# Attention, routed experts and a rational layer on one core: stage one reordered around the early gather, with its constants, fillers and weight splits moved

## The chip, the core and the metric

The kernel runs on one core of a Trainium2 chip. The core has a matrix engine (PE, TensorE; its weight loads are listed as PEld), a vector engine (DVE), a scalar engine (ACT), GpSimd (POOL), and SyncE (SP), which here only issues DMAs. The metric is the time of the program on the device in microseconds (us); lower is better.

## The reference, cut to what matters

Three layers follow each other.

1. **Decayed attention** (batch 2, 8 heads, 768 steps, head size 64): `state = gamma * state + k v^T; y = scale * q state`. Its output is read as `x`, 1536 tokens by 512.
2. **Routed experts** (8 experts, 512 to 1024 to 512, capacity 384 rows each): `logits = x @ w_gate`; each token goes to its `argmax` expert, at the next free position in arrival order; `h = max(x w1, 0)`, `y = h w2`, and the row is scaled by the softmax value of its expert.
3. **A rational layer** (512 to 2048 to 512): `h = x @ w_in`, `g = P(h) / (Q(h) + 1e-6)`, `out = g @ w_out`.

All is in single precision. The kernel gets this from a faster product by splitting each operand into a rounded high part and the rest ("split", H and L), and making three products of them.

## The kernel before, in words

**Stage one** handles 12 tiles of 128 tokens (`t` = 0 to 11, NT = 12; the first batch is t = 0 to 5). In `pe_tile(t)` PE transposes q and k of tile t+1, makes the gate products of tile t-1 (`pe_logits_apart`, `pe_logits_sum`), the state product, the row transposes (`pe_rows`), the query-state product, the scores of t+1, the positions of t-1 and last the values of t (`pe_values`). DVE in `dve_tile(t)` copies the gate sums, chooses the expert of each token (`dve_choose`), makes `tok_hot` (`dve_token`), turns the running count into a place (`dve_place`), masks the scores of t+1 (`dve_mask`), and at t = 6 to 9 takes one quarter of a weight split (`dve_split`, 128x1024). ACT copies results out of the banks and makes the high part of the split; POOL applies the decay tables; SP loads q, k, v three tiles ahead, stores each tile's rows to `xbuf` in memory (`store_x`) and loads weights. `pe_index(t)` adds a tile's tokens to the table of which token sits in which slot.

**The tail of stage one.** The first expert's rows must be in place before its first product. All but those of the last two tiles come by an early gather: once tile 9 is in the table, `dve_index0` copies the first 256 slots, and POOL issues two indirect DMAs from `xbuf` into `xd` (`pool_x_stored`). PE turns them (`pe_x_stored`, 8 products against the identity), and adds the rows of the last two tiles by products with a selection matrix (`pe_x_late(0)` and `(1)`, whose matrices come from `dve_fit`). ACT and DVE split the sum (`act_xH_first`, `dve_xL_first`), and `pe_up` of expert 0 starts. `act_gates` and `dve_gates` make the softmax values, which nothing needs before layer three. `pe_hold(n)` is n idle products of 128x128 on zeros.

**The experts and layer three** are long rows of products on PE, each weight matrix loaded (2 MB at a time) and split in turn.

The order on each engine is that of the code; engines meet only by semaphores. Each engine, and SP's list of DMAs, goes through its list in that order, and an instruction that waits holds up all behind it. The constants come as one table `cst` in four DMAs on ACT's queue, two under the semaphore `s_ident`, two under `s_cst`.

## Time and profile before

| what | us |
|---|---|
| median of 3 runs (lowest to highest) | 574.54 (572.18 to 575.68) |
| the profiled execution, its own time | 575.22 |
| its span in the trace | 573.4 |
| PE busy | 549.8 (96%) |
| DVE busy | 404.2 (70%) |
| ACT busy | 320.8 (56%) |
| stage one up to the first expert's product | 96.7 |

The span is cut by the hardware profiler around the engines' work; 1.8 us lie outside of it. In the profile a row names the line of the kernel, the engine, the operation and what it writes and reads.
### The profile page before, as it was taken

The numbers are of one execution on the slowest core, as the hardware profiler recorded it, in microseconds if no ns is written. First come the engines' busy times: TensorE is split into PE (matmuls) and PEld (weight loads), VectorE is DVE, ScalarE is ACT, GpSimd is POOL, SyncE is SP. The second block draws the span as 40 slices with busy tenths as digits, with TensorE's granted clock in tenths as the row PEclk, the third lists the DMA queues.
The fourth block names the chain that finished last, engine by engine and source line by source line (L and its number), as shares of the span: only waits on it lengthen the run. The fifth ranks groups of instructions, "written<-read, shape, count | busy, mean of one in ns | idle before, by whom it ended". The sixth has DMA issues, their size and how long they took to land.

```text
span 573.4 us, 9046 instructions
## 1 busy us (share of the span) xinstructions
PE 549.8 (96%) x3415; PEld 468.3 (82%) x3415; DVE 404.2 (70%) x718; ACT 320.8 (56%) x480; POOL 56.1 (10%) x55
## 2 busy tenths in 40 slices
PE   8999868999999999999958999999999999999997
PEld 6887757998989989989736888888888888888885
DVE  3567764745647457464758988888888888888885
ACT  3546421635646446454856757565775755756553
POOL 3424311101001011000050000100000000000000
PEclk9999998999999999999978999999999999999999
DMA  9999749367994583853040000100100000100001
GB/s 218 274 241 276 217 154 346 123 248 245 417 376 174 200 290 137 304 201 130 37 114 1 1 19 19 37 2 0 75 18 19 0 2 1 74 0 1 0 1 74
DMA packets 63871, 72.64 MB, mean 127 GB/s; under 512 B 39890, under 2 KB 40402, under 8 KB 63827
## 3 DMA queue, kind: packets, MB, share of 16 engines
q1 hardware_dynamic: 58706, 60.06, 31.6%
q0 software_dynamic: 2240, 7.34, 4.1%
q10 hardware_dynamic: 2880, 4.66, 2.2%
q8 instruction: 27, 0.44, 0.3%
q14 instruction: 18, 0.14, 0.1%
HBM read 59.20 MB, written 12.85 MB: 126 GB/s over the span
## 4 chain that ended last, share of the span: by engine, by line
PE 89%; DVE 4%; DMA 2%; ACT 2%; issue 1%; POOL 0%; POOLq 0%; DVEq 0%
PE bank L755 26%; PE bank L757 25%; PE bank L756 25%; PE bank L252 2%; PE bank L275 1%; DMA xd<-xbuf,index 1%; PE bank L286 1%; PE bank L719 1%; PE bank L1020 1%; DVE T L689 1%; PE bank L320 1%; PE bank L236 1%; DMA x2n<-ybuf,slot_all 1%; DVE atm L408 1%; PE bank L304 1%
## 5 line engine op out<-in xcount | busy, mean ns | idle before, releaser
L689 DVE TENSOR_TENSOR T<-raw,T 128x1024 fp32r<-128x1024 f32 x64 | 77.1, 1232 | 54.9 <-ACT T L683 54.6
L755 PE MATMUL bank<-x2H,T 128*128 128x512 f32 x192 | 76.8, 400 | 3.6 <-DVE pa L1108 2.2
L1078 ACT ACTIVATE sq<-bank 128x512 f32<-128x512 f32 x48 | 28.7, 597 | 86.1 <-PE bank L757 85.9
L757 PE MATMUL bank<-x2H,T 128*128 128x512 f32 x192 | 75.6, 394 | 0.0
L756 PE MATMUL bank<-x2L,T 128*128 128x512 f32 x192 | 75.5, 393 | 0.0
L755 PE MATMUL bank<-T,gL 128*128 128x512 f32 x192 | 74.8, 390 | 0.0
L757 PE MATMUL bank<-T,gH 128*128 128x512 f32 x192 | 74.7, 389 | 0.0
L756 PE MATMUL bank<-T,gH 128*128 128x512 f32 x192 | 74.7, 389 | 0.0
L755 PE MATMUL bank<-xH,T 128*128 128x256 f32 x256 | 72.5, 283 | 1.6 <-DVE xL L750 1.6
L756 PE MATMUL bank<-xL,T 128*128 128x256 f32 x256 | 72.5, 283 | 0.0
L757 PE MATMUL bank<-xH,T 128*128 128x256 f32 x256 | 72.5, 283 | 0.0
L683 ACT ACTIVATE T<-raw 128x1024 fp32r<-128x1024 f32 x64 | 65.2, 1058 | 4.6 <-ACT ysb L814 3.6
L1097 DVE SCALAR_TENSOR_TENSOR wa<-sq,coef,wa 128x512 f32<-128x512 f32 x48 | 36.0, 750 | 39.8 <-ACT wa L1080 39.8
L755 PEld LDWEIGHTS bank<-xH,T 128*128 128x128 f32 x256 | 49.1, 192 | 2.1 <-issue 1.8
L755 PE MATMUL bank<-T,hL 128*128 128x512 f32 x128 | 50.7, 396 | 0.0
L757 PE MATMUL bank<-T,hH 128*128 128x512 f32 x128 | 49.9, 390 | 0.0
L756 PE MATMUL bank<-T,hH 128*128 128x512 f32 x128 | 49.8, 389 | 0.0
L756 PEld LDWEIGHTS bank<-xL,T 128*128 128x128 f32 x256 | 49.1, 192 | 0.3
L757 PEld LDWEIGHTS bank<-xH,T 128*128 128x128 f32 x256 | 49.1, 192 | 0.0
L755 PEld LDWEIGHTS bank<-x2H,T 128*128 128x128 f32 x192 | 36.6, 191 | 12.1 <-issue 3.0
L757 PEld LDWEIGHTS bank<-x2H,T 128*128 128x128 f32 x192 | 36.5, 190 | 7.9
L756 PEld LDWEIGHTS bank<-x2L,T 128*128 128x128 f32 x192 | 36.6, 191 | 7.4
(139 smaller groups left out, 1023.0 us busy)
## 6 DMA issues: line engine op xcount, KB each, us to landing
raw<-in_moe_w_dram SPq DMA_DIRECT2D x14, 2048.0 KB, 10.5
raw<-in_moe_w_dram SPq DMA_DIRECT2D x8, 512.0 KB, 4.9
ybuf<-ysb ACTq DMA_DIRECT2D x16, 256.0 KB, 5.4
w_in_raw<-in_moe_w_in_dram SPq DMA_DIRECT2D x2, 2048.0 KB, 18.5
raw<-in_moe_w_out_dram SPq DMA_DIRECT2D x4, 1024.0 KB, 9.2
qin<-in_q_dram SPq DMA_DIRECT2D x12, 256.0 KB, 5.2
kin<-in_k_dram SPq DMA_DIRECT2D x12, 256.0 KB, 4.7
vin<-in_v_dram SPq DMA_DIRECT2D x12, 256.0 KB, 5.1
```

Source lines behind the costliest of these rows:

```text
L236: last = e.transpose(bank[0][:, p * P:(p + 1) * P], qs[t % 2][:, p * P:(p + 1) * P], ident)
L252: last = e.matmul(bank[2 + r][:, p * P:(p + 1) * P], kT[t % 2][rows, p, :], qT[t % 2][rows, p, :], start=True, stop=True)
L275: e.matmul(bank[4][:, p * P:(p + 1) * P], state[(t - 1) % 2][:, p, :], qT[t % 2][:, p, :], start=p == 0, stop=False, skip_group_check=True)
L286: last = e.matmul(bank[4][r * D:(r + 1) * D, p * P:(p + 1) * P], vs[t % 2][:, h * D:(h + 1) * D], atm[t % 2][:, r, p, :], start=t % C == 0 ...
L304: e.matmul(bank[7][:, 0:E], lgT[:, :], pick[:, :], start=True, stop=True).then_inc(s_lg, 1)
L683: e.activation(W[w][:, 0, cols], raws[par][:, w, cols], ACT.Copy).then_inc(r.wH[w], 1)
L689: e.tensor_tensor(W[w][:, 1, cols], raws[par][:, w, cols], W[w][:, 0, cols].bitcast(F32), ALU.subtract).then_inc(r.wL[w], 1)
L755: nc.tensor.matmul(out_, aL, bH, start=start, stop=False)
L756: nc.tensor.matmul(out_, aH, bL, start=False, stop=False)
L757: return nc.tensor.matmul(out_, aH, bH, start=False, stop=stop)
L1078: e.activation(sq[o][:, :], h[:, :], ACT.Square).then_inc(s_w, 1)
L1097: e.scalar_tensor_tensor(out=wa[n % 2][:, :], in0=sq[n % 2][:, :], scalar=coef[:, 5:6], in1=wa[n % 2][:, :], op0=ALU.mult, op1=ALU.add).th ...
```

## The change

- `dve_split` in stage one moves from the end of `dve_tile` (behind the mask) to between `dve_token` and `dve_place`.
- Tail on PE: the table product of tile 9 stands before the values of tile 10, not after them; that of tile 10 goes to the end. The positions of tile 10 come after the values of tile 11. `pe_x_late(0)` stands before `pe_x_stored` and starts the accumulation.
- Tail on DVE: `dve_index0` stands in tile 10 right behind `dve_place(9)`, before the mask of tile 11. In the last tile `dve_fit(1)` stands before `tok_hot`, `lane_hot` and `tok`.
- The first expert's split (`act_xH_first`, `dve_xL_first`) stands before the gate computations.
- SP: the 2 MB load of expert 1's first matrix moves from t = 9 to behind the last `store_x`, which itself waits for the early gather.
- Constants: three DMAs on ACT's queue (identity, decay tables, causal mask) and one on SP's behind the first six loads; `before` and `ones` are computed on DVE; the small tables are made behind the first two masks.
- Fillers: 8 to 5 at the start, 3 to 2 and 1 in the tail; the last 6 stay.

```diff
@@ dve_tables
-            e.wait_ge(s_cst, 16 * 2)
-            e.tensor_copy(before[:, :], cc("before")).then_inc(s_const, 1)
-            e.tensor_copy(ones[:, :], cc("ones")).then_inc(s_const, 1)
+            e.tensor_tensor(before[:, :], causal, ident, ALU.subtract).then_inc(s_const, 1)
+            e.memset(ones[:, :], 1.0).then_inc(s_const, 1)
...
+            e.wait_ge(s_cst, 16)
@@ dve_place(t, last=False)
             e.tensor_scalar(inside[:, :], step_no[:, :], step_of[:, :], None, ALU.is_equal).then_inc(s_in, 1)
+            if last:
+                dve_fit(1)
+                dve_token(t)
@@ pe_first_tile
-            pe_hold(8)
+            pe_hold(5)
@@ pe_tile
-            if t >= 2:
+            if t >= 2 and t != NT - 1:
                 pe_index(t - 2)
...
             if t + 1 < NT:
                 pe_scores(t + 1)
-            pe_positions(t - 1)
+                pe_positions(t - 1)
+                if t == NT - LAST:
+                    pe_index(t - 1)
             pe_values(t)
@@ pe_last_tiles
-            pe_index(NT - 2)
-            pe_hold(3)
+            pe_positions(NT - 2)
+            pe_hold(2)
             pe_logits(NT - 1)
             pe_rows(NT - 1)
+            pe_x_late(0)
+            pe_positions(NT - 1)
+            pe_hold(1)
             pe_x_stored()
-            pe_positions(NT - 1)
-            pe_x_late(0, False)
-            pe_x_late(1, True)
+            pe_x_late(1)
+            pe_index(NT - 2)
             pe_index(NT - 1)
@@ dve_tile
                 dve_token(t - 1)
+                if SPLIT_FROM < t <= SPLIT_FROM + WC:
+                    dve_split(main, 0, 0, 0, t - SPLIT_FROM - 1)
                 dve_place(t - 1)
+                if t == NT - LAST:
+                    dve_index0()
             if t + 1 < NT:
                 dve_mask(t + 1)
-            if SPLIT_FROM < t <= SPLIT_FROM + WC:
-                dve_split(main, 0, 0, 0, t - SPLIT_FROM - 1)
@@ sync
+            e.dma_start(cst[:, lay["kdecay"][1]:CW], consts[:, lay["kdecay"][1]:CW]).then_inc(s_cst, 16)
             e.wait_ge(s_zm, 2)
...
-                if t == NT - 3:
-                    sp_weights(main, 0, 1, 0)
             e.wait_ge(main.xd, 16 * NMAIN)
             store_x(NT - 1)
+            sp_weights(main, 0, 1, 0)
@@ scalar
             act_rows(NT - 1)
+            act_xH_first()
             act_gates()
@@ vector
             dve_first_q()
+            e.wait_ge(s_causal, 16)
+            dve_mask(0)
+            dve_tile(0)
             dve_tables(e)
...
             dve_fit(0)
             dve_choose(NT - 1)
-            dve_token(NT - 1)
-            dve_place(NT - 1)
-            dve_fit(1)
+            dve_place(NT - 1, True)
             dve_index()
+            dve_xL_first()
```

The next lists show the order of instructions on an engine at three places. `[waits ...]` names semaphores. First DVE in tile 6 of stage one, from `tok_hot` of tile 5 to the copy of the next gate sums. `T<-raw,T` is the split, `junk` and `cum` open the place computation, `atm` is the mask, and `lgT` is the copy that PE's gate sum waits for. Before:

```order
L443 TENSOR_SCALAR tok_hot<-hot_all,row_no 128x8 [waits s_hot]
L449 SCALAR_TENSOR_TENSOR junk,pt_all<-bank,hot_all 128x8 [waits s_ps]
L451 TENSOR_TENSOR cum<-cum,hot_all 128x8
L453 TENSOR_SCALAR junk,step_of<-step_at,pt_all 128x3 [waits s_pc]
L456 SCALAR_TENSOR_TENSOR lane_of<-step_of,pt_all 128x1 [waits s_so]
L458 TENSOR_SCALAR inside<-step_no,step_of 128x3
L461 TENSOR_SCALAR lane_hot<-cst,lane_of 128x128 [waits s_im,s_lo]
L464 TENSOR_TENSOR tok<-tok_hot,inside 128x24 [waits s_th,s_in]
L408 TENSOR_TENSOR atm<-bank,cst 128x512 [waits s_y,s_sc]
L408 TENSOR_TENSOR atm<-bank,cst 128x512
L689 TENSOR_TENSOR T<-raw,T 128x1024 [waits main_w1H]
L422 COPY lgT<-bank 128x128 [waits s_lg,s_la]
```

Now, the same place:

```order
L443 TENSOR_SCALAR tok_hot<-hot_all,row_no 128x8 [waits s_hot]
L698 TENSOR_TENSOR T<-raw,T 128x1024 [waits main_w1H]
L449 SCALAR_TENSOR_TENSOR junk,pt_all<-bank,hot_all 128x8 [waits s_ps]
L451 TENSOR_TENSOR cum<-cum,hot_all 128x8
L453 TENSOR_SCALAR junk,step_of<-step_at,pt_all 128x3 [waits s_pc]
L456 SCALAR_TENSOR_TENSOR lane_of<-step_of,pt_all 128x1 [waits s_so]
L458 TENSOR_SCALAR inside<-step_no,step_of 128x3
L464 TENSOR_SCALAR lane_hot<-cst,lane_of 128x128 [waits s_im,s_lo]
L467 TENSOR_TENSOR tok<-tok_hot,inside 128x24 [waits s_th,s_in]
L408 TENSOR_TENSOR atm<-bank,cst 128x512 [waits s_y,s_sc]
L408 TENSOR_TENSOR atm<-bank,cst 128x512
L422 COPY lgT<-bank 128x128 [waits s_lg,s_la]
```

The split stood in front of `lgT`; it now stands in front of `junk`, which waits for PE's positions (`s_ps`).

Second, PE at the end of tile 10: positions of tile 9 (L328, L329), values of tile 10 (L286), the table product (L341) and the gate product of tile 10 (L297). Before:

```order
L328 MATMUL bank<-hot_all,before 128x8 [waits s_lc,s_cum,s_hot]
L329 MATMUL bank<-cum,ones 128x8
L286 MATMUL bank<-atm,vs 64x128 [waits s_xT,s_mk,s_vs]
L286 MATMUL bank<-atm,vs 64x128 x7
L341 MATMUL bank<-tok,lane_hot 128x24 [waits s_se,s_ix]
L297 MATMUL bank<-xT,wg 32x128 [waits s_pc,s_xT]
```

Now:

```order
L328 MATMUL bank<-hot_all,before 128x8 [waits s_lc,s_cum,s_hot]
L329 MATMUL bank<-cum,ones 128x8
L341 MATMUL bank<-tok,lane_hot 128x24 [waits s_se,s_ix]
L286 MATMUL bank<-atm,vs 64x128 [waits s_xT,s_mk,s_vs]
L286 MATMUL bank<-atm,vs 64x128 x7
L297 MATMUL bank<-xT,wg 32x128 [waits s_pc,s_xT]
```

The table product, which waits for the end of `dve_place(9)` (`s_ix`), is now ahead of the values, and they wait behind it.

Third, PE from the last tile's row transposes (L320) on: L351 (L350 now) is `pe_x_stored`, L365 `pe_x_late`, L601 (L608) the count per expert, L222 a filler. Before:

```order
L320 MATMUL bank<-cst,xT 128x128 [waits s_x,s_xT]
L320 MATMUL bank<-cst,xT 128x128 x3
L351 MATMUL bank<-cst,xd 128x128 [waits s_mk,main_xd]
L351 MATMUL bank<-cst,xd 128x128 x7
L328 MATMUL bank<-hot_all,before 128x8 [waits s_lc,s_cum,s_hot]
L329 MATMUL bank<-cum,ones 128x8
L365 MATMUL bank<-fit,xt 128x256 [waits s_fit,s_x]
L365 MATMUL bank<-fit,xt 128x256 x3
L365 MATMUL bank<-fit,xt 128x256 [waits s_fit,s_x]
L365 MATMUL bank<-fit,xt 128x256 x3
L341 MATMUL bank<-tok,lane_hot 128x24 [waits s_ix]
L601 MATMUL bank<-cum,ones 128x8 [waits s_pc,s_cum]
```

Now:

```order
L365 MATMUL bank<-fit,xt 128x256 [waits s_mk,s_fit,s_x]
L365 MATMUL bank<-fit,xt 128x256 x3
L328 MATMUL bank<-hot_all,before 128x8 [waits s_lc,s_cum,s_hot]
L329 MATMUL bank<-cum,ones 128x8
L222 MATMUL bank<-zero 128x128
L350 MATMUL bank<-cst,xd 128x128 [waits main_xd]
L350 MATMUL bank<-cst,xd 128x128 x7
L365 MATMUL bank<-fit,xt 128x256 [waits s_mk,s_fit,s_x]
L365 MATMUL bank<-fit,xt 128x256 x3
L341 MATMUL bank<-tok,lane_hot 128x24 [waits s_index0,s_ix]
L341 MATMUL bank<-tok,lane_hot 128x24 [waits s_ix]
L608 MATMUL bank<-cum,ones 128x8 [waits s_pc,s_cum]
```

One of the two late products and the last positions now stand ahead of the wait for the gather (`main_xd`).

## Rows read from the trace of the kernel before

**Rows 1.** The chain that ended last, by engine, share of the span.

```profile
PE 89%; DVE 4%; DMA 2%; ACT 2%; issue 1%; POOL 0%; POOLq 0%; DVEq 0%
```

**Rows 2.** That chain in time, first 9 us: start us, us, what (x records).

```profile
3.54 3.41 PE bank L222 x16
6.96 0.62 PE bank L236 x4
...
8.83 1.16 PE bank L252 x16
```

**Rows 3.** Instructions in time, first 14 us: start us, us, engine, line [idle before].

```profile
5.11 0.69 DVE L532 TENSOR_TENSOR qs<-qin,cst 128x512 f32<-128x512 f32 x1 [2.46 <-DMA cst<-consts_dram]
...
11.97 1.04 POOL L532 TENSOR_TENSOR qs<-qin,cst 128x512 f32<-128x512 f32 x1 [0.41 <-DMA qin<-in_q_dram]
...
13.92 0.66 PE L236 MATMUL bank<-cst,qs 128*128 128x128 f32 x4
```

**Rows 4.** Stretches from:to: us, busy of PE, PEld, DVE, ACT, POOL, PEclk, DMA.

```profile
6.00:8.00 2.00, 2.00 (x13) 1.76 (x12) 0.70 (x6) 0.40 (x1) 0.43 (x1) 1.00 1.23 278
...
86.00:87.00 1.00, 0.81 (x4) 0.81 (x5) 0.00 (x0) 0.00 (x0) 0.00 (x0) 0.50 0.03 10
```

**Rows 5.** PE in time, tiles 7 to 10: gate sums that waited.

```profile
51.37 0.39 PE L304 MATMUL bank<-pick,lgT 128*128 128x8 f32 x2 [0.64 <-DVE lgT L422]
...
65.62 0.39 PE L304 MATMUL bank<-pick,lgT 128*128 128x8 f32 x2 [1.55 <-DVE lgT L422]
```

**Rows 6.** DVE and POOL in time, 42 to 72 us.

```profile
42.66 0.17 DVE L449 SCALAR_TENSOR_TENSOR junk<-bank,hot_all 128x8 f32<-128x8 f32 x1 [1.26 <-PE bank L329]
...
47.73 0.17 DVE L449 SCALAR_TENSOR_TENSOR junk<-bank,hot_all 128x8 f32<-128x8 f32 x1 [0.36 <-PE bank L329]
...
56.55 2.13 POOL L532 TENSOR_TENSOR qs<-qin,cst 128x512 f32<-128x512 f32 x1
...
63.49 1.87 DVE L689 TENSOR_TENSOR T<-raw,T 128x1024 fp32r<-128x1024 f32 x1
...
70.82 1.21 DVE L689 TENSOR_TENSOR T<-raw,T 128x1024 fp32r<-128x1024 f32 x1
```

**Rows 7.** The chain in time, end of stage one.

```profile
91.66 1.97 PE bank L365 x8
...
96.72 0.35 PE bank L755
```

**Rows 8.** Instructions in time, 75 to 95 us.

```profile
75.22 1.09 PE L286 MATMUL bank<-atm,vs 128*64 128x128 f32 x16
...
76.43 0.19 PE L341 MATMUL bank<-tok,lane_hot 128*128 128x24 f16 x1
...
77.49 0.15 DVE L484 CAST index<-bank 128x2 uint32<-128x2 f32 x1
...
77.89 0.39 PE L304 MATMUL bank<-pick,lgT 128*128 128x8 f32 x2 [0.45 <-DVE lgT L422]
...
79.78 1.09 PE L286 MATMUL bank<-atm,vs 128*64 128x128 f32 x16
...
79.92 0.95 POOL L709 DMA_INDIRECT xd<-xbuf,index  x1 [0.30 <-issue]
...
81.26 0.60 DVE L477 TENSOR_SCALAR fit<-cst,lane_of,mine 128x128 f32<-128x128 f32 x2
...
86.19 3.42 PE L351 MATMUL bank<-cst,xd 128*128 128x128 f32 x16 [2.82 <-DMA xd<-xbuf,index]
...
93.52 1.58 PE L222 MATMUL bank<-zero 128*128 128x128 f32 x12
```

**Rows 9.** The tile xd: landing of its 16 gathers, from their issue.

```profile
DMA to landing us min/median/max: 4.1/7.2/7.8
```

**Rows 10.** ACT in time: splits of expert 1's first matrix.

```profile
109.97 3.90 ACT L683 ACTIVATE T<-raw 128x1024 fp32r<-128x1024 f32 x4
```

More of the change, by code:

```diff
@@ L170, in build_program @@
         s_ident, s_cst, s_par, s_zm, s_const = (sem(n) for n in ("s_ident", "s_cst", "s_par", "s_zm", "s_const"))
-        s_wg, s_q0, s_xz, s_la, s_lt = (sem(n) for n in ("s_wg", "s_q0", "s_xz", "s_la", "s_lt"))
+        s_wg, s_q0, s_xz, s_la, s_lt, s_causal = (sem(n) for n in ("s_wg", "s_q0", "s_xz", "s_la", "s_lt", "s_causal"))
         s_index0, s_mine, s_fit, s_x0 = (sem(n) for n in ("s_index0", "s_mine", "s_fit", "s_x0"))
@@ L347, in pe_x_stored @@
             e.wait_ge(main.xd, NMAIN * 16)
-            e.wait_ge(s_mk, 2 * NT)
             for kk in range(KD):
@@ L351, in pe_x_stored @@
                     last = e.matmul(x_bank(kk)[:, s * P:(s + 1) * P], xd[:, s, kk * P:(kk + 1) * P], ident,
-                                    start=kk % 2 + s == 0, stop=False, skip_group_check=True)
+                                    start=False, stop=False, skip_group_check=True)
             last.then_inc(main.xt, NMAIN)
@@ L356, in x_bank, with pe_x_late @@
             return bank[2 + kk // 2][:, kk % 2 * NMAIN * P:(kk % 2 + 1) * NMAIN * P]
-        def pe_x_late(i, last_one):
+        def pe_x_late(i):
             e = nc.tensor
@@ L363, in pe_x_late @@
             e.wait_ge(s_fit, NMAIN * (i + 1))
+            e.wait_ge(s_mk, 2 * NT)
             for kk in range(KD):
                 last = e.matmul(x_bank(kk), xt[t % 2][:, kk * P:(kk + 1) * P], fit[i][:, :, :].rearrange("p a b -> p (a b)"),
-                                start=False, stop=True, skip_group_check=True)
-                if last_one and kk % 2:
+                                start=i == 0 and kk % 2 == 0, stop=i == LAST - 1, skip_group_check=True)
+                if i == LAST - 1 and kk % 2:
                     last.then_inc(s_x0, 1)
@@ L443, in dve_token, with dve_place @@
             e.tensor_scalar(tok_hot[t % 2][:, :], hot_all[:, t, :], row_no[:, t:t + 1], None, ALU.mult).then_inc(s_th, 1)
-        def dve_place(t):
+        def dve_place(t, last=False):
             e = nc.vector
@@ L859, in step @@
                     stored()
-            if split:
-                act_xH_first()
-            else:
+            if not split:
                 act_first_split(r)
@@ L877, in step @@
                         dve_split(r, *following(i, par), 0, c)
-            if split:
-                dve_xL_first()
-            else:
+            if not split:
                 for c in range(WC):
@@ L1347, in _ @@
         def _(e):
-            for a, b, s in ((0, lay["ident"][1], s_ident), (lay["qdecay"][0], lay["kdecay"][1], s_ident),
-                            (lay["ident"][1], lay["qdecay"][0], s_cst), (lay["kdecay"][1], CW, s_cst)):
+            for a, b, s in ((lay["ident"][0], lay["ident"][1], s_ident), (lay["qdecay"][0], lay["kdecay"][1], s_ident),
+                            (lay["causal"][0], lay["causal"][1], s_causal)):
                 e.dma_start(cst[:, a:b], consts[:, a:b]).then_inc(s, 16)
@@ L1394, in _ @@
             e.wait_ge(s_const, 6)
-            dve_mask(0)
-            for t in range(NT - 1):
+            for t in range(1, NT):
                 dve_tile(t)
-            dve_index0()
-            dve_tile(NT - 1)
             dve_fit(0)
             dve_choose(NT - 1)
-            dve_token(NT - 1)
-            dve_place(NT - 1)
-            dve_fit(1)
+            dve_place(NT - 1, True)
             dve_index()
+            dve_xL_first()
             e.wait_ge(s_cnt, 1)
```

## The prediction, on record before the change was run

> **What bounds the kernel now.** I read the chain of waits by engine first: PE holds 89% of it [rows 1], and from the first expert's product at 96.72 on it is one row of products, so what is taken off before 96.72 comes off the end one for one. The same chain in time order shows what PE does at the start: it sits in its own fillers [rows 2]. PE's instructions in time with their idle time show four late gate sums in tiles 7 to 10 [rows 5], and the tail shows PE waiting for the gather and then for the last split [rows 7, 8]. So there are three places, and I cost each. The profiled execution took 575.22 us, 0.7 above the median of the three runs, so the sum is made against 575.22.
>
> **Start.** 16 filler records take 3.41 us, 0.213 each [rows 2]; three fillers are six records, 1.28 us, and the rest would end at 5.68. The first decayed q is ready at 5.11 + 0.69 = 5.80 [rows 3], so the transposes could begin at 5.85 and not at 6.96: 1.1 us. PE's products still have the slow length there (the first of the transposes was the last slow one), so the 8 transposes up to 8.83 lose what they had as fast ones, about 0.4 to 0.5 us. The small tables on DVE are six operations, 0.70 us together [rows 4]; they stood in idle time and now stand between the second mask and PE's first gate product, beside PE's transposes of tile 2, 0.66 us for a group of four [rows 3]; I take 0.1 for what sticks out. The part of the constants that moves to SP is one more issue ahead of q of tile 2. Before, POOL waited 0.41 us for that q and was done at 13.01, and PE used it at 13.92 [rows 3]: 0.9 us of room, which the earlier start uses up, but there are also two tables fewer to fetch. I take **0.5 us** gained; the ends are 1.1 (all of it) and -0.3 (q of tile 2 late by one issue, and none of the filler time kept).
>
> **Middle.** PE waited for `lgT` four times behind a split: 0.64, three such waits, and 1.55 once [rows 5], 3.47 us in all. The split now fills the time in which DVE waits for the positions. In a full tile that is 1.26 us [rows 6], and a split is 1.21 [rows 6]: it fits, with no more than 0.05 to spare, in three tiles. In tile 6, which has no query-state product, the wait is only 0.36 [rows 6]. There the split pushes place and mask by 1.21 - 0.36, some 0.8 us, and they are next late for `lgT` of the following tile; before, the whole 1.21 stood there and made 0.64, so about 0.25 us is left. Gain 3.47 - 0.25 = **3.2 us**. The long wait of 1.55 belongs to a split that took 1.87 [rows 6]. In two other tiles POOL's decay took 2.13 beside the split [rows 6], where its others take 1.04 as in [rows 3]: the two disturb each other, and either can be the one that loses. In the new place POOL's decays are over, so I let the whole 1.55 go. The GPSIMD Engine Reference of the Trainium skill (section "Specifications") says that GpSimd shares its SBUF interfaces with VectorE and that vector instructions with two SBUF inputs contend; the trace agrees, by those 2.13 and 1.87. Ends: 3.5, and 1.6, where the 0.91 of excess comes back and 0.3 remains in each of the other tiles.
>
> **Tail,** in the times of the trace before. The table product of tile 9 stood at 76.43 and took 0.19 [rows 8]; the values of tile 10 now come behind it, at 76.62 and not 75.22: **1.4 us later**. From these values to the next was 79.78 - 75.22 = 4.56; the wait of 0.45 for `lgT` behind the mask [rows 8] mostly goes, since PE comes later: 4.1. So the values of tile 11 start at 80.7 and end at 81.8 (1.09). The positions of tile 10, which stood just ahead of them, are now behind. From the positions to the end of `fit` was 81.86 - 79.7 = 2.1 to 2.2 [rows 8]: 84.0. Until then PE has two fillers, the logits and the rows. Then `pe_x_late(0)`, 1.97 [rows 7], to 86.0, the positions and one filler to 86.5, and `pe_x_stored` can start, against 86.19 before: **0.3 later**.
>
> The gather need be there only then. Its copy of the index came at 77.49; it now follows the table product at once, at 76.7, 0.8 sooner, and the second gather, issued at 79.92 before [rows 8] and landed just ahead of PE's start at 86.19, 6.2 us later, is issued at 79.1. At that it lands at 85.3, at the longest of the sixteen, 7.8 [rows 9], at 86.9. The wait is about gone, whichever way. The 2 MB load ahead of it was no hindrance that I count, so I give its move nothing.
>
> `pe_x_stored` took 3.42 for 16 records, 0.214 each, at half the clock [rows 4, 8]; fillers at full clock take 1.58 / 12 = 0.13 [rows 8]. PE had been idle 2.8 us before it; that idle time is now filled, so I take 2.3 and not 3.42: **1.1 gained**. Behind it stood positions and `pe_x_late(0)`, 91.66 - 89.61 = **2.05, gone from there**. `pe_x_late(1)` then starts at 88.8.
>
> From the start of `pe_x_late(1)` to the first product was 96.72 - 91.66 = 5.06 [rows 7], with DVE's gate computations in between. Now the split follows at once: the sum ends 1.97 later, the index copy and the first low part need about 1.0 more, and PE's own last fillers end at 95.10 - 91.66 = 3.44 [rows 8]. The fillers are the later: 3.5 with the extra table product, **1.55 gained**. Tail: -0.3 + 1.1 + 2.05 + 1.55 = 4.4; I take **4.3**. The ends are 2.9 (the gather at its longest and `pe_x_stored` still at half clock) and 4.9.
>
> What is late next: the gate computations run on DVE during expert 0's first products, some 2 us of work in front of a split of its second matrix, which is needed only when all products of the first are made. Expert 1's first matrix is split on ACT from 109.97 on [rows 10], now some 4 us sooner, at 105.6; its load, issued at about 87, has over 18 us. Nothing there costs anything as long as that holds.
>
> **Sum:** 0.5 + 3.2 + 4.3 = 8.0 us; 575.22 - 8.0 = **567.2 us**.
>
> **Rivals.**
>
> *The split is not hidden.* The margin is 0.05 us in a wait of 1.26, and tile 6 has none. If each split still delays place, mask and `lgT` by 0.5 us on PE, the middle gives 1.0 and not 3.2: 569.4. Against it: 1.21 was measured beside nothing of POOL's, and that is how it will run. Chance 0.12.
>
> *The tail gives half.* The values of tile 10 wait behind the table product for DVE's place, and all that hangs on them moves. If that chain costs 2 us more than I have, or the gather lands as late as before for another reason, the tail gives 2 us: 569.5 to 570.5. For it: I have moved this chain over five instructions that wait for each other, and each term of it was read from another order of work. Chance 0.15.
>
> *The load behind the gather starves expert 1.* Three loads of 2 MB now leave one after the other, with expert 1's two gathers among them. If these took over 11 us, 3 more than the longest [rows 9], PE would wait at expert 1; 2 to 5 us, 569 to 572. Chance 0.04.
>
> *Slower: the half clock.* At the start and in the tail PE gets fewer fillers and a new wait of 1.1 us in front of the table product. The trace shows 0.50 granted right after an idle time of 2.8 us [rows 4, 8]. If the clock is at half from the table product to the first expert's products, `pe_x_stored` keeps its 1.1, the two late products take some 2 more, the other 7 us of PE work in the tail 3.5 more, the expert's first products 1.5, and a start that stays slow 2: 10 us against a gain of 8, **577**. It decides against the change from 8 us of such losses on. TensorE: Matmul & The Clock Gate of the Trainium skill (part 1, "The HAM clock gate") says that the throttled clock is the default and only activity releases it, which speaks against taking fillers away. By that rule this case is the likelier the emptier PE gets. The rows have PE fuller in the tail than before, so I give it 0.05.
>
> **The numbers.** Forecast 0.60 (565.5 to 569.0 by itself), the rivals 0.36, unforeseen 0.04. The lower ends of the terms, -0.3 + 1.6 + 2.9 = 4.2, give 571.0; the upper, 1.1 + 3.5 + 4.9 = 9.5, give 565.7. With 0.5 us for the spread of a median of such runs the range is 565.0 to 571.5; outside of it are the half clock, part of the starving and little else. A difference under 1%, 5.7 us, can hardly be told from none here; faster by more than that means under 568.8. The forecast nearly all lies there, the first two rivals hardly: faster 0.62, same 0.32, slower 0.06.
>
> **What would show it.** Right: no wait of PE for `lgT` in tiles 8 to 10 and about 0.25 in tile 7; every split at 1.2; `pe_x_stored` at about 2.3 us with a granted clock of 1.00, starting within 0.5 us of the end of its filler; the first expert's product at 88.5 to 89 on the trace's own time, right behind the last filler. Wrong: splits at 1.9, idle time of PE in front of `pe_x_stored`, 0.50 granted anywhere between 76 and 90, a wait of POOL for q of tile 2 of over 1 us, or PE idle at the start of expert 1.

## The result and the profile after

| | median us (lowest to highest, executions) | against the kernel before of the same session |
|---|---|---|
| before | 573.95 (572.18 to 576.63, 20) | |
| the change | 570.62 (566.47 to 573.37, 20) | 0.9932 (0.9913 to 0.9952) |

The change is 3.3 us faster, 0.7%. The profiled execution took 570.54 us, its span is 568.7, against 575.22 and 573.4. The forecast was 567.2 in a range from 565.0 to 571.5: the time is inside, but well under half of the forecast gain of 8.0 is there (4.7 us between the two profiled executions, 3.3 between the medians). The executions of the change spread over 6.9 us, those of the kernel before over 4.5 here and over 7.7 and 7.9 us in two later sessions of measurement, so it is not shown that the change spreads more.

**Where the time went.** These are the starts of PE's tiles (`pe_transpose_qk`) and the first product of expert 0, read from PE's instructions in time:

| | tile 2 | tile 6 | tile 7 | tile 8 | tile 9 | tile 10 | first product |
|---|---|---|---|---|---|---|---|
| before | 19.87 | 43.58 | 48.65 | 55.32 | 61.99 | 69.58 | 96.72 |
| the change | 20.06 | 43.77 | 48.84 | 58.31 | 64.27 | 70.23 | 91.12 |

(`pe_tile(n)` begins with the transposes of tile n+1; that is the time given.) The start lost 0.2. Tile 7 took 9.47 instead of 6.67 and gave back what tiles 8 (5.96 for 6.67), 9 (5.96 for 7.59) and 10 gained. So the positions of tile 9, which PE computes in tile 10, come at 75.03, and came at 75.08 before. From there to the first product it is 16.1 instead of 21.6, 5.55 us shorter. Of the 5.6 at the first product 5.5 are left at the last copy of the output (564.68 for 570.16) and 4.7 in the span, since the last rows took 0.8 longer to land.

Start of the change, instructions in time (start us, us, engine, line, operation, [idle before, releaser]); it answers to [rows 2, 3]:

```profile
6.21 0.63 PE L236 MATMUL bank<-cst,qs 128*128 128x128 f32 x4 [0.74 <-DVE qs L535]
...
8.10 1.16 PE L252 MATMUL bank<-qT,kT 64*128 64x128 f32 x16 [0.83 <-ACT kT L376]
...
13.90 1.04 POOL L535 TENSOR_TENSOR vs<-vin,cst 128x512 f32<-128x512 f32 x1 [0.91 <-PE bank L236]
13.92 1.04 DVE L206 TENSOR_SCALAR step_at<-cst 128x3 f32<-128x3 f32 x1
...
14.88 0.16 DVE L207 TENSOR_SCALAR step_no<-cst 128x3 f32<-128x3 f32 x1
...
15.13 0.43 PE L297 MATMUL bank<-xT,wg 128*32 128x128 f32 x8 [0.85 <-issue]
```

The scores begin at 8.10 and not 8.83: 0.73 gained. Then one of the small tables, 128 by 3, takes 1.04 us, where its twin of the same form and size takes 0.16 right behind. It began 0.02 us after POOL's decay and ended with it. PE's first gate product waits 0.85 for these tables (in the kernel it waits for `s_const`, which the last of them completes; the profile names no releaser).

Tile 7 in time: VectorE, then POOL, then PE:

```profile
47.47 1.22 DVE L698 TENSOR_TENSOR T<-raw,T 128x1024 fp32r<-128x1024 f32 x1
48.60 0.16 DVE L449 SCALAR_TENSOR_TENSOR junk<-bank,hot_all 128x8 f32<-128x8 f32 x1
...
49.14 1.02 DVE L458 TENSOR_SCALAR inside<-step_no,step_of 128x3 f32<-128x3 f32 x1
50.08 1.14 DVE L464 TENSOR_SCALAR lane_hot<-cst,lane_of 128x128 f16<-128x128 f32 x1
```

```profile
49.07 1.06 POOL L535 TENSOR_TENSOR vs<-vin,cst 128x512 f32<-128x512 f32 x1 [3.03 <-PE bank L286]
50.10 1.04 POOL L535 TENSOR_TENSOR qs<-qin,cst 128x512 f32<-128x512 f32 x1
```

```profile
51.37 0.19 PE L341 MATMUL bank<-tok,lane_hot 128*128 128x24 f16 x1 [1.43 <-DVE tok L467]
...
52.76 0.48 PE L304 MATMUL bank<-pick,lgT 128*128 128x8 f32 x2 [0.24 <-DVE lgT L422]
53.10 1.10 PE L320 MATMUL bank<-cst,xT 128*128 128x128 f32 x4
53.99 1.92 PE L275 MATMUL bank<-qT,state 128*128 128x128 f32 x8
```

The split is hidden, as forecast, and pushes the start of `dve_place` from 47.73 [rows 6] to 48.60, as forecast. What was not forecast: `inside` and `lane_hot` now meet POOL's two decays and take 1.02 and 1.14 where they take 0.22 and 0.28 in another tile (43.40 and 43.53). The row that PE waits for, `tok`, is late by that, and PE stands for 1.43 us. Stretches of one us (from:to, us, busy of PE, PEld, DVE, ACT, POOL, granted clock of PE, DMA share, GB/s):

```profile
50.00:51.00 1.00, 0.00 (x0) 0.00 (x0) 1.00 (x2) 0.68 (x2) 1.00 (x2) 1.00 0.80 236
51.00:52.00 1.00, 0.63 (x13) 0.42 (x15) 1.00 (x4) 0.00 (x0) 0.14 (x1) 1.00 1.04 304
...
53.00:54.00 1.00, 1.00 (x7) 1.00 (x7) 0.61 (x4) 0.35 (x1) 0.00 (x0) 0.50 0.94 213
54.00:55.00 1.00, 1.00 (x6) 1.00 (x6) 0.93 (x4) 0.76 (x2) 0.00 (x0) 0.50 1.14 262
55.00:56.00 1.00, 1.00 (x7) 0.78 (x5) 0.77 (x1) 0.78 (x1) 0.00 (x0) 0.50 0.52 160
```

Behind that wait 0.50 is granted, 1.2 GHz, from 53 to 56: the transposes L320 take 1.10 instead of 0.64, the query-state product 1.92 instead of 1.06. That is some 1.6 us on top of the wait. "TensorE: Matmul & The Clock Gate" of the Trainium skill (part 1) says that idle stretches of PE bring the throttled level back. These rows agree, with 0.50 behind a wait of 1.43, though waits in other tiles and runs did not bring it, as the experiments show.

The tail in time; it answers to [rows 7, 8]:

```profile
76.38 0.19 PE L341 MATMUL bank<-tok,lane_hot 128*128 128x24 f16 x1 [1.14 <-DVE tok L467]
76.50 1.09 PE L286 MATMUL bank<-atm,vs 128*64 128x128 f32 x16
...
78.29 0.43 PE L297 MATMUL bank<-xT,wg 128*32 128x128 f32 x8 [0.70 <-ACT xT L383]
...
79.06 0.95 POOL L718 DMA_INDIRECT xd<-xbuf,index  x1 [0.31 <-issue]
79.13 0.39 PE L304 MATMUL bank<-pick,lgT 128*128 128x8 f32 x2 [0.41 <-DVE lgT L422]
...
84.03 1.97 PE L365 MATMUL bank<-fit,xt 128*128 128x256 f32 x8
...
86.19 1.95 PE L350 MATMUL bank<-cst,xd 128*128 128x128 f32 x16
...
87.97 1.89 PE L365 MATMUL bank<-fit,xt 128*128 128x256 f32 x8
```

No wait in front of the gathered rows' product (L350), which takes 1.95 at a clock of 1.00 where it took 3.42 [rows 8]. The three waits of 1.14, 0.70 and 0.41 came with the new order. In this execution the clock held behind them.

### The profile page after: what moved, and what is told of

Read it like the earlier page. It is cut to its first block, busy times and chain, and to the rows that moved or that the text cites. A ratio compares the mean times of both kernels' runs of the same rounds, so it can differ in the third digit from the quotient of the medians.

```text
span 568.7 us, 9034 instructions
## 1 busy us (share of the span) xinstructions
PE 548.0 (96%) x3409; PEld 466.8 (82%) x3409; DVE 405.7 (71%) x718; ACT 321.9 (57%) x480; POOL 54.0 (9%) x55
## 4 chain that ended last, share of the span: by engine, by line
PE 92%; DVE 2%; DMA 2%; ACT 2%; issue 1%; POOL 0%; POOLq 0%; ACTq 0%; DVEq 0%
PE bank L764 26%; PE bank L766 26%; PE bank L765 26%; PE bank L252 2%; PE bank L286 2%; PE bank L275 2%; PE bank L236 1%; PE bank L728 1%; PE bank L320 1%; PE bank L1025 1%; PE bank L266 1%; DMA x2n<-ybuf,slot_all 1%; DMA cst<-consts_dram 1%; PE bank L241 1%; PE bank L304 1%
```

## The experiments

The theory after the two traces. **One:** a VectorE operation on SBUF data that begins beside POOL's decay is held until that ends, and the edits at the start and in tile 6 push short operations there. **Two:** the waits that this and the new tail give PE let the granted clock fall, in some executions here, in others there, and that takes back part of the gain. The main rival to both: the tail's new order is simply worth less than the trace of one execution shows.

The expectations below number their own theories, and "theory one" in them is not always One here. All medians below are also given against the kernel before of the same session (medians 575.2, 575.18 and 574.74 in the three sessions; 573.95 beside the change). The kernel before itself moves by 1.25 us between sessions, and the intervals are 2 to 5 us wide, so differences of 1 to 2 us between two experiments are not shown by the medians alone; for these the traces are read.

**e1_tail_only: the tail's part alone on the kernel before.** Start, constants and the place of the split are undone:

```diff
@@ dve_tile, of the change
-                if SPLIT_FROM < t <= SPLIT_FROM + WC:
-                    dve_split(main, 0, 0, 0, t - SPLIT_FROM - 1)
                 dve_place(t - 1)
...
                 dve_mask(t + 1)
+            if SPLIT_FROM < t <= SPLIT_FROM + WC:
+                dve_split(main, 0, 0, 0, t - SPLIT_FROM - 1)
@@ pe_first_tile
-            pe_hold(5)
+            pe_hold(8)
```

> Only the tail of the change on the kernel before: order on PE and DVE at the end of stage one, load of expert 1 behind the gather, split of the first rows ahead of the gate computations; splits of tiles 6 to 9, constants and the first 8 fillers as before. My theory (the tail gives all of the gain, and start and middle cancel out in sum): from the positions of tile 9 to the first product of expert 0 it takes 16.1 us as with the whole change and not 21.6; first product at 91.2, time 5.5 us under the kernel before, ratio 0.990. Rival (the tail's gain needs the PE time that the middle freed or lost): under 3 us.

Measured: 571.64 us (569.08 to 572.07), 3.6 below before, ratio 0.9925 (0.9899 to 0.9952). That is neither the 5.5 of the expectation nor the under 3 of its rival. First product at 92.73, 4.0 before the old 96.72. The same three waits stand in the tail, and here the clock falls behind them:

```profile
79.00:80.00 1.00, 0.73 (x4) 0.73 (x5) 0.31 (x2) 0.00 (x0) 0.80 (x1) 0.52 0.53 78
80.00:81.00 1.00, 1.00 (x6) 1.00 (x5) 0.85 (x5) 0.15 (x1) 0.15 (x1) 0.50 0.55 209
81.00:82.00 1.00, 1.00 (x7) 1.00 (x6) 0.23 (x1) 0.44 (x1) 0.00 (x0) 0.50 0.50 160
```

So the tail by itself makes about what the whole change makes, and in this execution it carries a loss of its own.

**e2_split_only: the place of the split alone on the kernel before.**

```diff
@@ dve_tile, of the kernel before
                 dve_token(t - 1)
+                if SPLIT_FROM < t <= SPLIT_FROM + WC:
+                    dve_split(main, 0, 0, 0, t - SPLIT_FROM - 1)
                 dve_place(t - 1)
```

> Only the move of the four splits between tok_hot and place, on the kernel before. My theory: tiles 8 to 10 lose their waits for lgT (0.64 + 1.55 + 0.64 = 2.8 us gained), but in tile 7 the place computation of tile 5, pushed by 0.9 us, runs beside POOL's decays; inside and lane_hot take about 1.0 and 1.1 us instead of 0.2 and 0.3, PE waits 1.4 us for tok, and the clock falls to half for some 3 us. Tile 7 then is 9.4 us and not 6.7: sum 0 (ratio 1.000, within 0.002). Rival A (as predicted before: tile 6 costs 0.25 only): 3.2 us gained, 0.994. Rival B (the half clock comes from the fillers taken away at the start): tile 7 waits 1.4 but stays at full clock, 1.8 us gained, 0.997.

Measured: 572.45 us (569.95 to 573.88), 2.8 below before, ratio 0.9933 (0.9905 to 0.9962). The expectation of no gain was wrong. The three later tiles take 5.96 each, as forecast. Tile 7 takes 7.0: `inside` 1.02 beside POOL's first decay, `lane_hot` only 0.27, since POOL's second decay waited for its q until 51.18. PE waited 0.56 and the clock held in this tile. (It fell later, behind the old wait for the gather, here 3.09 us long, for 6.8 us; before it was 3.4 us behind 2.82. So the first product of this execution is only 1.8 us earlier.) The middle is worth nearly its 3.2 where only one of the two operations is held and the clock stays up. The two gains, 3.6 and 2.8, don't add up to the change's 3.3. The product of their ratios is 0.9859, against 0.9932 (0.9913 to 0.9952) measured for the change.

**e3_split6_back and e4_split6_tables: the split of tile 6 back behind the mask; and the small tables ahead of the first tile's choice too.**

```diff
@@ dve_tile
-                if SPLIT_FROM < t <= SPLIT_FROM + WC:
+                if SPLIT_FROM + 1 < t <= SPLIT_FROM + WC:
                     dve_split(main, 0, 0, 0, t - SPLIT_FROM - 1)
...
                 dve_mask(t + 1)
+            if t == SPLIT_FROM + 1:
+                dve_split(main, 0, 0, 0, 0)
@@ VectorE's list, e4 only
             dve_mask(0)
+            dve_tables(e)
             dve_tile(0)
-            dve_tables(e)
```

> The whole change, with the split of tile 6 alone put back behind the mask (tiles 7 to 9 keep the new place). My theory: tile 7 is 6.7 us again, its gate sum waits 0.64 for lgT, and no half clock there: 2.8 us less than the whole change, about 8.3 less than before, ratio 0.9865 against 0.9932. Rival (the three others would show the same conflict with POOL, or the half clock comes from elsewhere): the same time as the whole change, 0.993.

> As the run before, and the small tables are made between the first and the second mask (DVE and POOL idle there), not behind the second, where step_at took 1.04 us beside POOL's decay and PE's first gate product waited 0.85. My theory: that wait is gone, tile 2 starts at 19.1 to 19.2 and not at 20.06; 0.85 us less than the run before, ratio 0.985. Rival (the table of constants that now comes on SP's queue lands after 11 us and holds the second mask up): nothing gained or a loss of up to 1 us, with DVE waiting for the DMA of cst.

Measured: e3 571.46 us (567.83 to 572.55), 3.7 below before, 0.992 (0.9888 to 0.9952); e4 569.42 (566.55 to 573.45), 5.8 below, 0.9892 (0.9845 to 0.9938). Both are less than the expectations, 0.9865 and 0.985; e3 is nearer to its rival of no gain, and the intervals of e3, e4 and the change overlap. In e3 tile 7 is 6.67 again and the first product comes at 90.54, but the same collision has moved to tile 8, where it costs nothing, and to tile 9, which takes 6.99 us. VectorE and, below it, POOL:

```profile
57.94 1.11 DVE L432 SCALAR_TENSOR_TENSOR rankv<-lg_all,mx_all,cst 128x8 f32<-128x8 f32 x1
...
61.36 1.02 DVE L458 TENSOR_SCALAR inside<-step_no,step_of 128x3 f32<-128x3 f32 x1
```

```profile
57.98 1.04 POOL L535 TENSOR_TENSOR qs<-qin,cst 128x512 f32<-128x512 f32 x1 [1.60 <-DMA qin<-in_q_dram]
61.30 1.05 POOL L535 TENSOR_TENSOR vs<-vin,cst 128x512 f32<-128x512 f32 x1 [2.27 <-PE bank L286]
```

In e4 PE's wait for the tables is gone: from the first scores to tile 2 it takes 11.04 us, as in the kernel before, and 11.83 in e3. Tile 2 itself begins at 19.50 and at 19.66 in e3, hardly earlier, because the first transposes of this execution took 1.09 and not 0.63. Both show half clock in the tail, e3 for 3.4 us, e4 for 6.8:

```profile
75.00:76.00 1.00, 0.32 (x8) 0.20 (x8) 0.36 (x1) 0.60 (x1) 0.98 (x1) 0.85 0.00 0
76.00:77.00 1.00, 0.59 (x10) 0.26 (x3) 0.29 (x1) 0.00 (x0) 0.69 (x2) 0.50 0.28 45
...
81.00:82.00 1.00, 1.00 (x13) 0.67 (x9) 0.00 (x0) 0.05 (x1) 0.00 (x0) 0.50 0.00 0
```

**e5_tail_fill: e4, with fillers where PE waits in the tail.** This is the direct test of Two.

```diff
@@ pe_tile, of e4
                 pe_positions(t - 1)
                 if t == NT - LAST:
+                    pe_hold(4)
                     pe_index(t - 1)
...
+            if t == NT - 1:
+                pe_hold(2)
             pe_logits_apart(t - 1)
             if t % C < C - 1:
                 pe_state(t)
+            if t == NT - 1:
+                pe_hold(1)
             pe_logits_sum(t - 1)
```

> The kernel of e4_split6_tables with seven fillers (128x128, about 0.21 us each) put where TensorE waited in the tail: four ahead of the table product of tile 9, two ahead of the gate product of tile 10 and one ahead of its sum; the waits there were 1.14, 0.70 and 0.41 us. Theory one, the half clock decides: the holes of 1.1 and 0.7 us are what lets the granted clock fall to 0.50 between 75 and 83 us in e4 (7 us long). With fillers the clock stays 1.00 there, each product keeps its time of full clock, and the first product of expert 0 comes about 1.5 to 2.5 us earlier (89 instead of 91.1); median 567.0 to 568.0, against 569.4. Theory two, the clock falls for another reason or where the half clock lies costs nothing on the path: fillers change nothing, or cost what they overshoot (0 to 0.3 us); median 569.4 to 569.8.

Measured: **567.12 us (566.86 to 568.39)**, 8.1 below before, ratio 0.9879 (0.9849 to 0.991). First product at 87.80 instead of 91.11; no stretch below full clock before the experts; the spread is 1.5 us instead of e4's 6.9. PE in time, and stretches of two us:

```profile
73.07 0.19 PE L341 MATMUL bank<-tok,lane_hot 128*128 128x24 f16 x1
73.19 1.09 PE L286 MATMUL bank<-atm,vs 128*64 128x128 f32 x16
74.21 0.71 PE L222 MATMUL bank<-zero 128*128 128x128 f32 x4
74.98 0.42 PE L297 MATMUL bank<-xT,wg 128*32 128x128 f32 x8
75.33 0.49 PE L222 MATMUL bank<-zero 128*128 128x128 f32 x2
75.82 0.39 PE L304 MATMUL bank<-pick,lgT 128*128 128x8 f32 x2
```

```profile
74.00:76.00 2.00, 1.95 (x22) 1.20 (x19) 0.95 (x3) 0.60 (x1) 1.37 (x2) 1.00 0.00 0
76.00:78.00 2.00, 2.00 (x22) 1.88 (x23) 1.18 (x6) 0.60 (x1) 0.70 (x1) 1.00 0.63 164
```

By the medians, seven fillers of no use to the result make the kernel 2.3 us faster. By the ratios, against the kernel before of each session, it is 0.7 us, with overlapping intervals of six executions each, so the size is open. The cause can be read more firmly. First in the traces, by the time from the start of tile 10 to the first product of expert 0:

| | waits in the tail | half clock in it, us | from tile 10 to the first product |
|---|---|---|---|
| before | old order, 2.82 for the gather | 3.4 | 27.14 |
| e1, e3, e4 | 1.14, 0.70, 0.41 | 3.4, 3.4, 6.8 | 23.06, 22.47, 23.49 |
| the change, e6, e8 | 1.14, 0.70, 0.41 | 0 | 20.89, 20.88, 20.88 |
| e5, e10 | filled | 0 | 20.88, 20.89 |

The fillers themselves cost nothing, and the half clock costs 1.6 to 2.6 us where it comes. That also answers the main rival: the new order is worth what the trace of the change shows wherever the clock holds. Second, each execution has a mean granted clock on record, in which 3.4 us at half clock are 0.003. (Every profiled execution, before and after, has another 10.2 or 13.7 us of half clock near 290 us, so the mean is not of the tail alone.) Without the fillers (the change, e1, e3, e4) it is 0.985 or less in 17 of 46 executions; with them (e9, e12, e10, e5) in 1 of 25. Two holds for the tail. The clock is not all of the spread, though: the 9 executions of the change at 0.990 or more have a median of 568.81 and the 11 others of 571.38, and 4.3 us of spread are left within the first group.

**e6_pool_short: the whole change, POOL's decay of tiles 6 to 10 on 2 of 8 heads** (the rest is left out).

```diff
@@ pool_decay and decayed, of the change
-            decayed(e, t, 2).then_inc(s_vs, 1)
+            decayed(e, t, 2, 2 if 6 <= t <= 10 else H).then_inc(s_vs, 1)
```

> The whole change, with POOL's decay of q and v cut to 2 of its 8 heads in tiles 6 to 10 (the rest keeps what the buffer held, so part of the result is left out): POOL's tensor_tensor there falls from 1.04 to some 0.3 us. Theory one, VectorE's short operations are held for as long as a POOL operation runs beside them: in tile 7 the operations inside (1.02) and lane_hot (1.14) fall back to about 0.22 and 0.28, the wait of 1.43 us ahead of the row that waits for tok goes to 0.2 or less, tile 7 takes 6.0 us instead of 9.5 and tiles 8 to 10 stay at 6.0; the profiled run then stands 3 us better by the first product of expert 0 (88), and the median falls by 0.5 to 3 us, by how many executions had the half clock there. Theory two, those two operations are slow by their own kind or place in the row: they stay at 1.0 and 1.1 us, the wait stays, and the median stays at 570.6.

Measured: 569.45 us (567.37 to 573.55), 5.7 below before, 0.9913 (0.9881 to 0.9944). POOL and VectorE in the same tile:

```profile
49.12 0.42 POOL L535 TENSOR_TENSOR vs<-vin,cst 128x128 f32<-128x128 f32 x1 [3.66 <-PE bank L286]
```

```profile
49.20 0.38 DVE L458 TENSOR_SCALAR inside<-step_no,step_of 128x3 f32<-128x3 f32 x1
49.49 0.27 DVE L464 TENSOR_SCALAR lane_hot<-cst,lane_of 128x128 f16<-128x128 f32 x1
```

The edit shortened `vs` alone (the decay of q kept its 8 heads, contrary to what the expectation says), and that suffices here: `inside` ends within 0.05 us of POOL's end again, now after 0.38. PE's wait for `tok` is gone (0.24 for `lgT` is left), and the tile takes 6.36. `lane_hot` met no decay in this execution, since POOL's second waited for its q until 50.70, so this run tests `inside` alone. Theory one of the expectation holds: the length of the hold-up is what is left of POOL's operation. Other runs say the same: `row_no` (128 by 12) began 0.17 us behind a decay of 1.04 in e3 and took 0.90, and 0.20 us behind one in e10 and took 0.86, 0.16 alone. The gain in the median, 1.2 us under the change, is within the noise.

**e7_two_inputs: the whole change, `inside` and `lane_hot` in the form with a second SBUF input.**

```diff
@@ dve_place, of the change
-            e.tensor_scalar(inside[:, :], step_no[:, :], step_of[:, :], None, ALU.is_equal).then_inc(s_in, 1)
+            e.scalar_tensor_tensor(out=inside[:, :], in0=step_no[:, :], scalar=step_of[:, :], in1=ONES,
+                                   op0=ALU.is_equal, op1=ALU.mult).then_inc(s_in, 1)
```

(`ONES` stands for a slice of the table of ones; `lane_hot` likewise. The third DMA of the constants is made longer, to fetch that table.)

> The whole change, with inside and lane_hot made by scalar_tensor_tensor with a second input (a table of ones in SBUF) instead of tensor_scalar, same sizes (128x3 and 128x128). If the hold-up beside POOL's decay belongs to the one-input form tensor_scalar, the new ones take 0.25 and 0.35 us beside it and tile 7 takes 6.0 us; the median falls by 0.5 to 3 us. If any VectorE operation that begins beside POOL's decay is held, they take 1.0 to 1.1 us where they meet it, as before, tile 7 takes 9.5 (7 where the clock holds) and the median is 570.6 or 0.1 us more per tile for the longer form (571.5).

Measured: 571.36 us (568.56 to 575.81), 3.8 below before, 0.9949 (0.992 to 0.9978). VectorE, then POOL:

```profile
49.49 1.01 DVE L458 SCALAR_TENSOR_TENSOR inside<-step_no,step_of,cst 128x3 f32<-128x3 f32 x1
50.42 0.34 DVE L466 SCALAR_TENSOR_TENSOR lane_hot<-cst,lane_of 128x128 f16<-128x128 f32 x1
...
50.78 1.28 DVE L408 TENSOR_TENSOR atm<-bank,cst 128x512 f32<-128x512 f32 x2
```

```profile
49.42 1.06 POOL L538 TENSOR_TENSOR vs<-vin,cst 128x512 f32<-128x512 f32 x1 [3.02 <-PE bank L286]
50.76 1.04 POOL L538 TENSOR_TENSOR qs<-qin,cst 128x512 f32<-128x512 f32 x1 [0.27 <-DMA qin<-in_q_dram]
```

The hold-up does not hang on the one-input form. `lane_hot` fell between the two decays here and took 0.34, so PE waited 0.63, the clock held, and the tile took 7.07. And the mask, which began 0.02 us after POOL's second decay, kept its 1.28: one of its two inputs comes from PSUM.

**e8_bulk_back: the whole change, the bulk load back at t = NT - 3.**

```diff
@@ SP's list, of the change
+                if t == NT - 3:
+                    sp_weights(main, 0, 1, 0)
             e.wait_ge(main.xd, 16 * NMAIN)
             store_x(NT - 1)
-            sp_weights(main, 0, 1, 0)
```

> The whole change, with the bulk load of expert 1's weights back in tile 9 of the loop on SP's queue (sp_weights at t = NT - 3) instead of behind the wait for the gather. Theory one (that of the prediction): the load's place costs and gives nothing; the gather lands by its own latency of 3.4 to 8.2 us, TensorE does not wait for it, and the median stays at 570.6 (570.0 to 571.2). Theory two: the load beside the gather delays its rows; the stored rows' product at 86 us then waits 1 to 3 us, expert 0 begins that much later, median 571.6 to 573.6.

Measured: 570.67 us (568.46 to 571.87), 4.5 below before, 0.9922 (0.9891 to 0.9953). The median is that of the change (570.62), the intervals overlap, and PE does not wait in front of the gathered rows' product (86.64, right behind its filler): no worth of the load's place shows. Tile 7 again has the wait of 1.43 and half clock behind it (9.46 us).

**e9, e10 and e12: the same fillers on the whole change, on e3 and on e1. e11: e5 with four fillers ahead of expert 0 instead of six** (`pe_hold(6)` to `pe_hold(4)` in `pe_last_tiles`).

> The whole change, nothing undone, with the seven fillers of e5_tail_fill in the tail's waits. Theory one: the place of the split in tile 6 and the half clock there are a loss of their own (tile 7 at 9.5 us in the profiled run of the change, 7.0 where the clock holds), the tail's half clock another. The fillers take away only the second: median 568.0 to 569.5, between the change (570.6) and e5 (567.1), and the profile shows tile 7 at 7 to 9.5 us and no half clock after 70 us. Theory two: the tail's half clock was all of it, and the split's place costs nothing in most executions: median 567.1 to 567.6.

> The kernel of e5_tail_fill with the constant tables back behind the first tile's choice on VectorE (as in the change), so that only their place differs from e5. Theory one, the tables' place costs what the gate product of tile 1 waits in the profiles (0.7 to 0.85 us, 1.7 in one): median 567.7 to 568.2. Theory two, the later rows absorb it (TensorE waits for the choice in every tile): median 567.0 to 567.3.

> The kernel of e5_tail_fill with four fillers instead of six ahead of expert 0's first product. In e5 the six end at 87.80 while xL's first half is written by 87.4 at the latest: two fillers fewer bring the first product 0.3 to 0.4 us earlier, median 566.7 to 566.8 (theory one). Rival: the product then waits for the second half of xL (written at about 88.0), and nothing is gained: 567.1.

> The kernel before with the change of the tail alone (that of e1_tail_only) and the seven fillers in its waits. Theory one: the new order of the tail is worth 5.5 us at full clock in the profiles and its half clock takes 2 to 3 of it back in e1 (571.6 against 575.2). With the fillers the median is 568.8 to 569.8, 5.5 to 6.5 below the kernel before, and the granted clock is 1.00 from 75 to 83 us. Theory two: the new order itself is worth no more than the 3.6 us that e1 measured, whatever the clock: median 571.3 to 571.9.

| | median us (lowest to highest) | ratio (interval) | below before: without and with the tail's fillers |
|---|---|---|---|
| e9, the change | 569.54 (566.59 to 572.73) | 0.9905 (0.9872 to 0.9938) | 3.3, 5.2 |
| e10, of e3 | 567.96 (566.95 to 569.97) | 0.989 (0.9864 to 0.9916) | 3.7, 6.8 |
| e12, of e1 | 570.17 (568.99 to 573.38) | 0.9928 (0.99 to 0.9956) | 3.6, 4.6 |
| e5, of e4 | 567.12 (566.86 to 568.39) | 0.9879 (0.9849 to 0.991) | 5.8, 8.1 |
| e11 | 566.92 (566.46 to 568.18) | 0.9865 (0.9841 to 0.9889) | with four last fillers: 7.8 |

By the medians the fillers help on all four bases, by 1.0 to 3.0 us; by the ratios on three (0.9932 to 0.9905, 0.992 to 0.989, 0.9892 to 0.9879) and not on e1 (0.9925 to 0.9928), with every pair of intervals overlapping. What they do to the clock is plain, what that is worth on each base is not.

e9 is 1.6 us slower than e10 of the same session, which would be the price of the split of tile 6; with 7 and 6 executions and overlapping intervals that is not shown. In e9's trace tile 7 takes 7.00 (6.67 in e10), there is no half clock before the experts, and PE loses 1.06 us elsewhere: in tile 6 its gate product waits for `xT`, which stands behind ACT's part of the split. In this execution the small tables met no hold-up either, and PE did not wait for them.

e10 against e5 gives 1.3 us for the tables' place against their own sessions, 0.8 by the medians as they stand. That is where theory one of e10 put it, the intervals overlap, and the traces give the same size: from the first scores to tile 2 it is 11.79 in e10 and 11.04 in e5.

e12 met neither expectation; in its profile the tail's clock is 1.00, but 0.50 is granted from 66 to 69, right behind the old wait of 1.56 us for the split at 65.17, which that kernel still has. So probably a part of its gain was taken there. e11 is as fast as e5 and the fastest of all, but 0.2 us apart is less than these runs can tell. Its own profiled execution, 568.18, had another collision in tile 8 (PE waits 0.44 for `tok`); from tile 10 to the first product it takes 20.67, 0.21 less than e5.

## Why the prediction came out as it did

**Start, forecast +0.5, traced -0.2.** The step that failed: "The small tables on DVE are six operations, 0.70 us together; I take 0.1 for what sticks out". Their time was read where nothing of POOL's ran. In the new place one meets a decay and takes 1.04. PE waits 0.85 (0.69 in e10, 1.68 in e8, nothing in e9). Going back on this edit made the traced start 0.8 us shorter each time (e3 to e4, e10 to e5); the medians fell by 2.0 and by 0.8 to 1.3, within the noise. The filler term came out in size: the scores began 0.73 earlier, where 1.1 less 0.4 to 0.5 was forecast. But the reason was another. The constants landed 0.26 later (q ready at 5.37, not 5.11), and the first transposes were not slow (0.63); in e4 and e5, with 1.09, they were.

**Middle, forecast +3.2, traced +0.25.** The waits for `lgT` in the three later tiles went, as forecast, and every split took 1.22. The step that failed: "In tile 6 ... about 0.25 us is left". The delay of `dve_place` was sized right (0.87), but it was priced only by what follows on VectorE; what POOL does at the same time was not looked at. I had written "In the new place POOL's decays are over", which is so for the splits and not for the operations that they push. "SBUF — State Buffer" of the Trainium skill (section "Who interferes with whom") has the mechanism: a VectorE operation with two SBUF inputs, or in a mode that uses both ports, and one of POOL's that reads SBUF exclude each other, and the one that issues first holds the other up for its whole length. Rows here agree, by 1.04, 1.02 and 1.14 beside 1.04 to 1.06, and by the mask's undisturbed 1.28; no row shows in which mode the operations with one input ran. In the profiled execution this and the half clock behind it cost 3.0 us; in e2, where only one operation was held and the clock stayed up, tile 7 took 7.0 and not 9.47.

**Tail, forecast +4.3, traced +5.55.** The chain up to `pe_x_late(0)` came out to 0.03 us (84.03 against 84.0). The rest was better: the stored rows' product started 0.3 sooner and left the path after 1.78, not 2.3, and the first product came 3.15 behind `pe_x_late(1)`, not 3.5. But that is an execution whose clock held. What I gave 0.05, as an all-or-nothing case of 10 us, happens in part in many executions: 6.8 us at half clock in e4's tail, 3.4 in those of e1 and e3, at a cost of 1.6 to 2.6 us. The rival named the right place, "a new wait of 1.1 us in front of the table product", and the wrong size. "The rows have PE fuller in the tail than before" was true of the sum (PE busy for 86% of 75 to 91.1 us, 73% of 75 to 97 before), but it did not keep the clock up: the three new waits all end within 3 us.

**The rivals.** The time fell just above where two rivals lay (569.4 and 569.5 to 570.5), by neither's mechanism: the splits were hidden and the tail gave all. The load behind the gather starved nobody (e8). That e5 has just the forecast gain, 8.1 of 8.0 (7.0 by its ratio), is partly chance, since its tail is better than in the sum and its tile 6 is that of the kernel before.

**The range** held by its lower ends (571.0), and by luck. The sum was made against 575.22, 1.3 above the median of the 20 executions beside the change. From 573.95 the same working ends at 570.2, and 570.62 lies outside. The chances should have given "within 1%" more than 0.32: two side effects that each take 1 to 3 us in a part of the executions.

What stays open: what decides in which execution the clock falls. The waits of 1.14, 0.70 and 0.41 left it at 1.00 in the profiles of the change, e6 and e8 (and 1.21, 0.70 and 0.41 in e7), and brought 0.50 in e1, e3 and e4. The 2.0 us between the medians of e3 and e4 are more than the 0.8 of the wait, and whether the rest is clock or noise is not known. And 4 us of spread at the same clock have no cause shown; the collisions that come and go between executions (`row_no`, `lane_hot`, `xT` in e9) are a candidate.

## What to carry to other kernels

When an operation on VectorE is moved, lay POOL's instructions beside its new place and beside the place of everything that it pushes: operations of 0.2 us became 1.0 here. When an order is changed so that PE gains a wait of about 1 us, try fillers of that length in it, and judge them by the time and granted clock of many executions, not by one trace. And price the parts of a change on a base without the others' side effects: here 3.6 and 2.8 alone, 3.3 together, and 8.1 (7.0 by the ratio) with the split of tile 6 and the tables back and the tail filled.

## What the runs showed of the hardware

- A VectorE operation of 128 by 3 with SBUF inputs takes 0.16 to 0.22 us alone and 1.01 to 1.04 beside POOL's decay of 1.04 to 1.06; beside one of 0.42 it takes 0.38. The form (one or two SBUF inputs) made no difference (1.01 in e7); an operation with an input from PSUM is not held (1.28 both ways).
- Not every operation beside POOL is held. In e9 one of the same 128 by 3 tables began 0.03 us behind POOL's decay and took its 0.16, and the decay took 1.09:

```profile
13.68 1.09 POOL L535 TENSOR_TENSOR vs<-vin,cst 128x512 f32<-128x512 f32 x1 [0.78 <-PE bank L236]
13.71 0.16 DVE L207 TENSOR_SCALAR step_no<-cst 128x3 f32<-128x3 f32 x1
```

- A granted clock of 0.50 came after single waits of 1.43 us (the change, e8), 1.56 (e12), 2.82 (before) and 3.09 (e2), and after groups of 1.14, 0.70 and 0.41 us (e1, e3, e4). It lasted 6.8 us in e2 and e4 and 3.4 in the others. It did not come in every execution: 1.55 and 1.56 (before, e1) and the same groups in the change, e6 and e8 left it at 1.00. Waits of 0.56 and 0.63 in tile 7 (e2, e9, e7) left it there too.
